# Moving the rounding of the second-layer weights in ScalarE's and GpSimd's orders of a fused attention and mixture-of-experts kernel

## The reference

```python
logits = x @ w_gate
logits = logits - logits.max()
P = np.exp(logits)
for _ in range(8):
    P /= P.sum(1, keepdims=True) + 1e-09
    P /= P.sum(0, keepdims=True) + 1e-09
    P *= N / E
out = np.zeros((N, D), dtype=np.float32)
for e in range(E):
    h = np.maximum(x @ w1[e], 0.0)
    ye = h @ w2[e]
    out += P[:, e:e + 1] * ye
```

## Time and profile before

| | us |
|---|---|
| median of 3 runs (1878.3 to 1879.43) | 1878.8 |
| the profiled execution | 1878.12 |
| its span, first to last instruction | 1876.3 |
| mean granted TensorE clock, as a share of 2.4 GHz | 0.998 |

### The profile page before, as it was taken

One profiled execution on the slowest core, in us unless ns is written; L12 is line 12 of the kernel. 1 busy time (PEld: TensorE's weight loads), 2 busy tenths in 40 slices (PEclk: granted clock), 3 DMA queues, 4 the chain that ended last, 5 costly groups with the idle time before them and its releaser, 6 DMA issues.

```text
span 1876.3 us, 28109 instructions
## 1 busy us (share of the span) xinstructions
PE 1844.5 (98%) x10255; PEld 1595.6 (85%) x10255; DVE 978.4 (52%) x1846; ACT 830.1 (44%) x1410; POOL 1059.5 (56%) x720
## 2 busy tenths in 40 slices
PE   8999999999999999999999999999999999999999
PEld 4677777688988999999998879999999999999998
DVE  8877777667643444346445534443444344434442
ACT  8776777533333333334333333333333333333331
POOL 0223325557666666666676566666666666666660
PEclk9999999999999999999999999999999999999999
DMA  7754462011111111112111111221221111111110
GB/s 245 221 147 95 122 150 66 27 65 68 68 68 68 68 68 68 68 68 101 68 67 68 68 67 53 71 71 71 72 103 68 68 68 68 68 68 68 68 46 34
DMA packets 44162, 152.56 MB, mean 81 GB/s; under 512 B 9594, under 2 KB 18042, under 8 KB 29710
## 3 DMA queue, kind: packets, MB, share of 16 engines
q1 hardware_dynamic: 44046, 151.04, 24.9%
HBM read 135.69 MB, written 15.34 MB: 80 GB/s over the span
## 4 chain that ended last, share of the span: by engine, by line
PE 91%; DVE 2%; issue 2%; ACT 1%; POOL 1%; DVEq 0%; ACTq 0%; POOLq 0%
PE banks L673 14%; PE banks L674 14%; PE banks L672 14%; PE banks L640 12%; PE banks L644 12%; PE banks L642 12%; PE banks L555 4%; PE banks L516 3%; PE banks L498 3%; PE banks L499 2%; PE banks L581 1%; PE banks L526 0%; DVE probs L1035 0%; POOL w_lo L1280 0%; DVE u L1164 0%
## 5 line engine op out<-in xcount | busy, mean ns | idle before, releaser
L1280 POOL TENSOR_TENSOR w_lo<-stage,w_hi 128x1024 fp32r<-128x1024 f32 (+1 forms) x288 | 645.5, 2255 | 524.7 <-ACT w_hi L842 523.4
L842 ACT ACTIVATE w_hi<-stage 128x1024 fp32r<-128x1024 f32 (+1 forms) x288 | 272.8, 978 | 510.9 <-PE banks L674 499.2
L674 PE MATMUL banks<-w_hi,h_lo 128*128 128x512 f32 x1152 | 450.1, 391 | 0.0
L673 PE MATMUL banks<-w_lo,h_hi 128*128 128x512 f32 x1152 | 449.9, 391 | 0.0
L672 PE MATMUL banks<-w_hi,h_hi 128*128 128x512 f32 x1152 | 448.9, 390 | 0.0
L1164 DVE TENSOR_TENSOR u<-p_copy,banks 128x384 f32<-128x384 f32 x192 | 106.3, 553 | 636.4 <-PE banks L644 631.0
L889 ACT ACTIVATE h_hi<-corner 128x384 fp32r<-128x384 f32 x384 | 202.0, 526 | 267.1 <-DVE corner L1164 264.0
L640 PE MATMUL banks<-x_hi,w_hi 128*128 128x384 f32 x896 | 302.8, 338 | 4.2 <-DVE u L1164 2.6
L644 PE MATMUL banks<-x_hi,w_lo 128*128 128x384 f32 x896 | 300.9, 336 | 0.0
L1170 DVE SCALAR_TENSOR_TENSOR h_lo<-corner,h_hi 128x384 fp32r<-128x384 f32 x384 | 295.0, 798 | 0.0
L674 PEld LDWEIGHTS banks<-w_hi,h_lo 128*128 128x128 f32 x1152 | 216.2, 188 | 45.2
(11 more groups left out here) (135 smaller groups left out, 2451.5 us busy)
## 6 DMA issues: line engine op xcount, KB each, us to landing
stage<-in_expert_w SPq DMA_DIRECT2D x96, 1024.0 KB, 4.7
raw<-in_qk SPq DMA_DIRECT2D x32, 576.0 KB, 7.2
bias_scratch<-bias_out SPq DMA_DIRECT2D x36, 288.0 KB, 2.8
bias<-bias_scratch SPq DMA_DIRECT2D x16, 288.0 KB, 2.8
v_main<-in_v SPq DMA_DIRECT2D x16, 256.0 KB, 2.6
bias<-bias_scratch SPq DMA_DIRECT2D x16, 256.0 KB, 3.8
out<-total SPq DMA_DIRECT2D x4, 768.0 KB, 3.8
out<-total SPq DMA_DIRECT2D x6, 256.0 KB, 2.0
```

Source lines behind the costliest of these rows:

```text
L673: pe.matmul(dst, h_hi[:, g % 2, f, tokens], lo[:, f], start=False, stop=False)
L674: mm = pe.matmul(dst, h_lo[:, g % 2, f, tokens], hi[:, f], start=False, stop=fp == FPAIRS - 1 and f == 1)
L842: act.activation(hi, of, ACT.Copy).then_inc(w_rounded, 1)
L1280: pool.tensor_tensor(lo, of, hi.bitcast(F32), ALU.subtract).then_inc(w_split, 1)
```

## The change

In ACT's order `round_weights` part 2 moves from the end of period g (for g + 2) to behind the first relu of period g + 1 (for the same weights, now called g + 1 there). The factor in advance (`round_factor`) is put ahead of parts 0 and 1 of g + 2. In period 0 nothing is rounded for period 2 at the end any more; that is done in the middle of period 1, in the same places in which period 0 rounds for period 1. In period 31 (`after == 1`) the factors 4 and 5 of the next token group stand apart. POOL's order follows: the sums of g + 2 stand first, then part 2 of g + 1, then parts 0 and 1 of g + 2; in periods 0 and 1 parts 0 and 1 of the next period stay ahead of the sums. PE, DVE and SP keep their code.

```diff
@@ ACT, loop over g @@
                 round_hidden(g, 0)
-                if after == 1:
-                    for k in range(4, 6):
-                        round_factor(1, k)
-                if g == 0:
-                    round_weights(1, 0)
+                if g < 2:
+                    round_weights(g + 1, 0)
+                elif more:
+                    round_weights(g + 1, 2)
                 if g == 2:
                     act.wait_ge(top_neg, 1)
                     act.activation(routing[:], routing[:], ACT.Exp, bias=top[:, 1:2]).then_inc(exp_ready, 1)
-                if g == 0:
-                    round_weights(1, 1)
+                if after == 1:
+                    round_factor(1, 4)
+                if g < 2:
+                    round_weights(g + 1, 1)
                 round_hidden(g, 1)
-                if g == 0:
-                    round_weights(1, 2)
+                if after == 1:
+                    round_factor(1, 5)
+                if g < 2:
+                    round_weights(g + 1, 2)
                 round_hidden(g, 2)
                 round_hidden(g, 3)
                 if after == 1:
                     round_factor(1, 6)
-                if g + 2 < ALL:
-                    for i in range(NW):
-                        round_weights(g + 2, i)
                 if at in IN_ADVANCE.get(p + 1, {}):
                     round_factor(p + 1, IN_ADVANCE[p + 1][at])
+                if 0 < g < ALL - 2:
+                    for i in range(2):
+                        round_weights(g + 2, i)
@@ POOL, loop over g @@
                 p, at = g // PERIODS, g % PERIODS
-                for i in range(NW):
-                    if g + 1 < ALL:
+                if g < 2:
+                    for i in range(2):
                         split_weights(g + 1, i)
                 if g + 2 < ALL:
                     sum_weights(g + 2)
+                if g + 1 < ALL:
+                    split_weights(g + 1, 2)
+                if 0 < g < ALL - 2:
+                    for i in range(2):
+                        split_weights(g + 2, i)
                 if 4 <= at < 4 + SUMS and p + 1 < TILE_PAIRS:
                     sum_factor(p + 1, at - 4)
```

## The result

The changed kernel takes 1865.96 us (median of 4 runs, 1865.77 to 1866.31) against 1878.82 (4 runs, 1878.3 to 1879.43): ratio 0.9932, 95% interval 0.9914 to 0.9949. It is faster by 12.9 us where 18.8 were forecast; the upper end of the forecast range is 1866. The profiled execution took 1865.84.

A forecast was written before the change was run, and what follows sets the result against it. PE, busy 98% of the span, was taken as the bound. Stalls -16.3, periods 0 and 1 -5.3, normalization +2.8: -18.8 us, giving 1860 us for the median; range 1855.5 to 1866.

The forecast's parts named there:

- the eight stalls: Waits of about 2.03 us in the periods right behind the eight of `IN_ADVANCE`; all to go: -16.3 us.
- periods 0 and 1: PE's gap around 366 us goes (-3.0) and the half clock behind it (-2.3): -5.3 us.
- rival 1: Period 1: the clock falls all the same, from narrow gate matmuls and transposes; 1862.3 us, chance 0.13.
- the block of the first rest: DVE's first rest of a period, held by POOL's split of part 2, ends near +7.1, 1.9 us late; PE loses 0.
- The chain of small steps in period 5: DVE's normalization steps that tile 4's side matmul waits for, blocked by POOL's splits; +0.6 us in period 5.
- Period 31: Factors 4 and 5 one relu earlier, DVE's three last rests still against POOL's two splits; 0, at most +0.5 us.
- rivals 3, 4 and 5: 3: half of each stall stays, 1872, 0.05; 4: DVE overruns add periods, 1885, 0.04; 5: copy still late, 1879, 0.03.
- Rival 4: In 23 add periods the first rest's block carries to the end and delays `u2`: +25, 1885 us, chance 0.04.
- the normalization: Periods 1 to 7: DVE's chain ends later behind POOL's later splits, delaying PE; +2.8 us, bounds -0.6 and +8.6.
- All that is read by PE in the next period or later: 0.: POOL's splits of parts 0 and 1 start 1.15 us later in each period; claimed to cost PE 0.
- the four tiles 4: Side matmuls waiting for DVE's normalization: +1.0 us in period 3, +0.6 each in 5 and 6, +0.3 in 2.
- four tiles 0: Side matmuls at tile 0 in the normalization periods: 0.1 us later at each of the four, or the like.

The follow-up runs named there:

- e1: The kernel before, with only the factor in advance put ahead of all three weight parts: 1863.02 us.
- e2: The changed kernel with part 2 back at the period's end and POOL's sums back behind all three splits, from period 2 on: 1856.69 us.
- e8: The changed kernel with POOL's sums straight behind the split of part 2, ahead of the other two splits, from period 2 on: 1867.5 us.
- e7: The changed kernel with DVE's first rest of a period behind the fourth corner instead of the second: 1865.47 us.
- e6: The changed kernel with the scaling of the first expert's total cut from 512 to 8 columns a tile: 1862.58 us (one run).
- e10: e8 with DVE's third and fourth rest behind the normalization of tile 4 in periods 2, 3, 5 and 6: 1859.78 us.
- e9: The changed kernel with the edits of e8 and e7 together: 1867.87 us.
- e11: The changed kernel with the DVE edit of e10 alone, POOL's order as changed: 1864.2 us.

## Why the prediction was right, and where it was wrong

**Right: the eight stalls.** Forecast -16.3, measured -16.24. The factor's place alone did it, as e1 shows: not the second layer's weights, but the factor behind them made `u2` late.

**Right: periods 0 and 1.** Forecast -5.3, measured -5.80, and -4.7 against e1, which has the old order too. All nine traces with the new order have 33.48 to 33.50. The gap went, and with it the half clock; the windows show 1.00 where the earlier trace rows had 0.86 and 0.55, so rival 1 is out.

```profile
366.00:371.00 5.00, 5.00 (x32) 4.75 (x31) 1.11 (x2) 2.16 (x8) 2.06 (x1) 1.00 0.33 108
```

It is 0.1 short of the far bound (-5.9), in which the transposes too had run at half.

**Right: the block of the first rest, and that it costs nothing in a steady period.** Forecast: end near +7.1; measured 912.49 + 2.40 - 907.86 = +7.03. The chain of small steps in period 5 was to end 0.6 later; it ends 447.86 - 433.83 = +14.03 behind the copy's start, before 449.45 - 436.00 = +13.45. Period 31 costs nothing (its stretch, 279.15, is 18 x 15.51).

**Right: that rivals 3, 4 and 5 would not come.** No stall is left by halves; from period 9 on the periods in which outputs are added keep their 15.51; and the order did what it says. Rival 4's mechanism, DVE overrunning its period by the blocks of its rests, did occur, but once and in another place: period 7, not the 23 add periods.

**Wrong: the normalization**, +2.8 forecast, +9.1 measured; the bounds (-0.6 to +8.6) just miss it. The total lies just inside its range only because the range had room for rivals that did not come; that is luck, and says nothing for this term. Period 8, too, was to be 15.51 and took 18.19. What I had costed is right in sum: the side matmuls at the four tiles 4 are later by 0.99, 0.77, 0.35 and 0.36 us in periods 2, 3, 5 and 6 and those at four tiles 0 by 0.12 each, together 2.95 for 2.8 (as written the forecast's terms add up to 2.9; period 2 was too low, 0.3, and periods 5 and 6 too high, 0.6 each). The step that failed is this one: "All that is read by PE in the next period or later: 0." It is true of the weights that POOL makes, and I let it stand for POOL's instructions. I had the sums in their right place, behind the splits (+13.6 to +16.6 forecast; +13.5 to +16.4 in the steady period above), but asked only when ACT needs them, not what they hold up on DVE. I followed the chain to the side matmul and stopped. Behind it in DVE's line stand the third and the fourth rest, the reading of the totals that the next first product waits for, and in period 7 six scalings; and on POOL the sums, which the change moves from the first half of the period to right behind the splits, so that POOL is busy exactly there. These waits are 0.36, 0.07, 1.16 and 1.16 us at the first products behind periods 2, 3, 5 and 6 and 2.55 at the fourth product of period 8: 5.3. With the 2.95 that makes 8.25 of the 9.1; the rest I did not place wait by wait.

Had that term been 9.1, the sum would have been -16.3 - 5.3 + 9.1 = -12.5, against -12.9 measured. That the term comes with the moved part 2 and the sums' place is shown by e2; the place of the sums alone doesn't give it back (e8). That it goes by POOL instructions met on DVE is borne out by the count of steps given with the theory, by e7 (two grew to three), by e6 (8 columns, 1.81 us) and by e10, where the waits that the theory said would go did go, though not its sum. ACT's and POOL's parts of the move were not taken apart.

On what blocks what, the Trainium skill ("SBUF — State Buffer", Who interferes with whom) says that a DVE step with two SBUF inputs and a GpSimd step that reads SBUF hold a shared port for whole instructions, that `tensor_scalar` can be one of those that need it, and that `tensor_reduce` never is. The traces agree: 2.40 for 0.55, 1.81 for 0.23, and reduces of 0.41 to 0.42 beside any POOL work.

## What to carry to other kernels

When a step is moved on one engine, list for the stretch where it lands every instruction of the neighbours that can't run beside it, by their order in line, and count the blocks one by one; here a delay in us was the wrong unit, and the number of instructions met the right one. Follow a chain past the place where it first reaches the bounding engine, to the last instruction of that period on each engine that feeds it. And split a change into its parts before keeping it: here two moved lines and a new order of two periods held all of the gain, and the moved part 2, most of the change, only a loss.

## What the runs showed of the hardware that was not expected

PE's clock did not always do the same behind equal waits. In e8 three first products waited alike (2.48 to 2.49 us from one matmul's start to the next, at the end of periods 3, 5 and 6). Behind the first and the third the clock fell, behind the second it didn't. The same three waits in e9 (2.66 to 2.67 us) went the same way. Windows of e8, from the end of the second wait and from that of the third:

```profile
452.02:454.02 2.00, 2.00 (x12) 2.00 (x13) 1.79 (x7) 0.49 (x1) 0.00 (x0) 1.00 0.00 0
...
470.50:474.90 4.40, 4.40 (x17) 4.40 (x18) 2.42 (x8) 0.49 (x1) 0.00 (x0) 0.65 0.00 0
```

In e11 a gap of 2.35 us in period 8 was followed by 5 us at 0.66, while the 2.72 us of the changed kernel, at the same product, were followed by 5 us at 1.00. Period 8 of e11 took 19.36 us, where 15.51 and the gap's 2.18 over the usual 0.17 come to 17.69: such a stall cost 1.7 us more here, and nothing more in the changed kernel (18.19, where 15.51 and 2.55 come to 18.06). What decides between the two was not tried.

The block goes both ways: beside DVE's scalings in period 7, POOL's two splits took 4.65 us in the changed kernel and 4.93 in e6, 4.20 in period 5, and the sums of 0.73 took up to 1.05.
